# Token-number copies moved behind the weight loads of the last stage, and one register load replaced by an addition

## The reference, cut to what matters

```
x = attention(q, k, v, w_phi)                    # [2304, 512]
e = argmax(x @ w_gate); gate = softmax(...)[e] * sigmoid(x @ w_output_gate)[e]
x = gate * (relu(x @ w1[e]) @ w2[e])             # hidden width 1024
xn = x / sqrt(mean(x*x) + 1e-6) * rms_g
out = (silu(xn @ w_g) * (xn @ w_val)) @ w_out    # hidden width 1536
```

## Time and profile before

| | |
|---|---|
| median of 3 runs | 903.44 us (901.85 to 903.90) |
| profiled execution, its own time | 900.01 us |
| its span | 898.3 us |
| PE matmuls busy | 875.0 us, 97% of the span |
| PE weight loads busy | 794.5 us, 88% |
| DVE, ACT, POOL busy | 430.7, 294.0, 123.0 us |
| experts' steps | about 211 to 436 us |
| FFN | about 436 to 896 us |

### The profile page before, as it was taken

One profiled execution on the slowest core, in us unless ns is written; L12 is line 12 of the kernel. 1 busy time (PEld: TensorE's weight loads), 2 busy tenths in 40 slices (PEclk: granted clock), 3 DMA queues, 4 the chain that ended last, 5 costly groups with the idle time before them and its releaser, 6 DMA issues.

```text
span 898.3 us, 16710 instructions
## 1 busy us (share of the span) xinstructions
PE 875.0 (97%) x6432; PEld 794.5 (88%) x6433; DVE 430.7 (48%) x875; ACT 294.0 (33%) x479; POOL 123.0 (14%) x145
## 2 busy tenths in 40 slices
PE   8999999999999999999899999999999999999996
PEld 6776859588999999999899999999999999999996
DVE  5688888997587434443456422222222222222222
ACT  4555545652356333222444321121121112112111
POOL 1010203033234221125200010010000001001001
PEclk9999999999999999999999999999999999999998
DMA  8614614021754444328633720030020002000000
GB/s 280 201 54 176 225 53 158 2 81 40 256 149 119 80 79 65 69 30 183 153 128 119 178 88 1 1 106 1 1 70 35 0 25 80 0 0 36 1 1 36
DMA packets 37185, 75.37 MB, mean 84 GB/s; under 512 B 8176, under 2 KB 24688, under 8 KB 35472
## 3 DMA queue, kind: packets, MB, share of 16 engines
q1 hardware_dynamic: 32832, 56.07, 23.5%
q0 software_dynamic: 3488, 17.85, 5.4%
q10 hardware_dynamic: 816, 0.79, 0.3%
HBM read 51.06 MB, written 23.64 MB: 83 GB/s over the span
## 4 chain that ended last, share of the span: by engine, by line
PE 85%; DVE 8%; issue 3%; ACT 2%; DMA 1%; POOL 0%; DVEq 0%; POOLq 0%; SPq 0%; ACTq 0%
PE ps L1025 11%; PE ps L1027 10%; PE ps L1026 10%; PE ps L1040 5%; PE ps L1041 5%; PE ps L1039 5%; PE ps L927 4%; PE ps L928 4%; PE ps L929 4%; PE ps L940 3%; PE ps L942 3%; PE ps L941 3%; PE ps L768 3%; PE ps L823 2%; PE ps L728 2%
## 5 line engine op out<-in xcount | busy, mean ns | idle before, releaser
L1025 PE MATMUL ps<-xnH,blkH 128*128 128x384 f32 x576 | 194.6, 338 | 3.3 <-DVE blkL L1692 2.3
L1027 PE MATMUL ps<-xnH,blkL 128*128 128x384 f32 x576 | 194.2, 337 | 0.0
L1026 PE MATMUL ps<-xnL,blkH 128*128 128x384 f32 x576 | 194.1, 337 | 0.0
L1699 DVE TENSOR_TENSOR sg<-sg,ps 128x384 f32<-128x384 f32 x72 | 39.9, 554 | 246.6 <-ACT sg L1258 246.6
L1258 ACT ACTIVATE sg<-ps 128x384 f32<-128x384 f32 x72 | 35.4, 491 | 253.2 <-PE ps L1027 253.2
L1025 PEld LDWEIGHTS ps<-xnH,blkH 128*128 128x128 f32 x576 | 108.8, 189 | 7.5 <-issue 4.7
L1026 PEld LDWEIGHTS ps<-xnL,blkH 128*128 128x128 f32 x576 | 108.9, 189 | 2.7
L1027 PEld LDWEIGHTS ps<-xnH,blkL 128*128 128x128 f32 x576 | 108.8, 189 | 0.0
L1040 PE MATMUL ps<-blkL,hH 128*128 128x512 f32 x216 | 84.9, 393 | 0.0
L1041 PE MATMUL ps<-blkH,hL 128*128 128x512 f32 x216 | 84.8, 393 | 0.0
L1039 PE MATMUL ps<-blkH,hH 128*128 128x512 f32 x216 | 84.6, 391 | 0.0
(11 more groups left out here) (219 smaller groups left out, 1552.5 us busy)
## 6 DMA issues: line engine op xcount, KB each, us to landing
stage<-in_ffn_w SPq DMA_DIRECT2D x12, 768.0 KB, 4.3
xin<-xs_dram SPq DMA_DIRECT2D x9, 578.2 KB, 9.9
xs_dram<-zrow SPq DMA_DIRECT2D x8, 578.2 KB, 8.0
qT<-in_q SPq DMA_DIRECT2D x4, 1152.0 KB, 6.5
xnH_dram<-xoH SPq DMA_DIRECT2D x8, 576.0 KB, 3.5
xnL_dram<-xoL SPq DMA_DIRECT2D x8, 576.0 KB, 4.9
xnH<-xnH_dram SPq DMA_DIRECT2D x6, 768.0 KB, 4.9
xnL<-xnL_dram SPq DMA_DIRECT2D x6, 768.0 KB, 6.3
```

The lines of the kernel that those rows point to most:

```text
L1025: e.matmul(o, hi, xnH[par][:, c, :], start=(c == 0), stop=False)
L1026: e.matmul(o, hi, xnL[par][:, c, :], start=False, stop=False)
L1027: last = e.matmul(o, lo, xnH[par][:, c, :], start=False, stop=(c == KC - 1))
```

## The change

In SP's program `rows_out` is cut in two. The stores of the rows stay; the copy of the token numbers becomes `numbers_out`, with the load of the row number that only it needs. In the loop it is called right behind `rows_out`. For the last two steps both copies stand behind the loads of all weight blocks and behind the last step's row stores, ahead of the wait for `xst` and of `group_in(1)`. In `over_turns` the first step of a pair's second turn is the sum of the first turn's two numbers, in place of a load.

```
+        def tiles_of(e, x):
+            return e.value_load(tab[0:1, bass.ds(x + TILES, 1)], min_val=0, max_val=NTOK // G)
...
-                    tiles, first = turn_of(e, pair * 2 + par)
+                    if par == 0:
+                        tiles, first = turn_of(e, pair * 2)
+                    else:
+                        first = first + tiles
+                        tiles = tiles_of(e, pair * 2 + 1)
...
             def rows_out(n):
-                col, row = column_of(n), row_of(n)
+                col = column_of(n)
                 e.wait_ge(s["act_xh"], n + 2)
...
                 e.dma_start(xnL_dram[:, :, bass.ds(col, G)], xoL[:, :, :].bitcast(F32)).then_inc(s["xst"], 16)
+
+            def numbers_out(n):
+                col, row = column_of(n), row_of(n)
                 e.wait_ge(s["idst"], n * 16 + 16)
                 settle(e, "carry_sp")
                 with nc.allow_non_contiguous_dma(reason="token numbers"):
...
             with e.Fori(0, total - 2) as n:
                 rows_next(n + 2)
                 rows_out(n)
+                numbers_out(n)
             rows_next(total)
...
             for i in range(3, NF):
                 block_in(i)
             rows_out(last)
+            numbers_out(prior)
+            numbers_out(last)
             e.wait_ge(s["xst"], total * 32 + 64)
             settle(e, "carry_sp")
             group_in(1)
```

More of the change, by code:

```diff
@@ L345, in piece_of, with tiles_of @@
             return w1[:, n, :] if n < KC else w2[:, 2 * (n - KC):2 * (n - KC) + 2, :].rearrange("p c n -> p (c n)")
+        def tiles_of(e, x):
+            return e.value_load(tab[0:1, bass.ds(x + TILES, 1)], min_val=0, max_val=NTOK // G)
         def turn_of(e, x):
-            tiles = e.value_load(tab[0:1, bass.ds(x + TILES, 1)], min_val=0, max_val=NTOK // G)
+            tiles = tiles_of(e, x)
             first = e.value_load(tab[0:1, bass.ds(x + FIRST, 1)], min_val=0, max_val=NTOK // G + E)
```

## The result

| | kernel before | changed kernel |
|---|---|---|
| median | 903.31 us (901.85 to 903.90, 4 runs) | 913.44 us (912.52 to 914.60, 4 runs) |
| ratio to before | | 1.011, 95% interval 1.0094 to 1.0126 |
| profiled execution, its own time | 900.01 us | 914.60 us |
| its span | 898.3 us | 913.0 us |

The change makes the kernel 10.1 us slower. I had forecast 4.0 us slower, with a range up to 910.0: the direction was right, the size was not, and the time lies above the range. In the lines of the changed kernel L1025 to L1027 of before are L1040 to L1042, L1692 is L1707, L533 is L546, L513 is L526, L498 is L510 and L518 is L531.

A forecast was written before the change was run, and what follows sets the result against it. PE was taken as the bound, 85% of the chain. Block 2 -3.7, register loads -1.0, stall +7.0 and clock +1.7 summed to +4.0 us, from a median of 903.44 to 907.4 us, range 900.5 to 910.0.

The forecast's parts named there:

- Part 3: Loop: row number loaded between stores and copy delays copy and `xin` load about 1.1 us, hidden by transposes; cost nothing.
- part 1: Block 2's load without a copy ahead lands earlier: 1.98 us of PE idling and 1.70 of slow clock go, gain 3.7.
- Part 4: Both copies ahead of group 1's rows: PE stalls 7.0 us, plus 1.7 us of slow clock behind it.
- (b): Bound on group 1's stall: row stores' own transfer is part of the first copy's time; rows land 520.6, stall 5.5 us.
- rival 3: Block 2's load is late because of the seam's row stores, not the copy; stall stays, +7.7, 911.1 us; chance 0.06.
- Part 2: Load of `first` goes twice on PE, ahead of the second and empty fourth turns: gain 1.0 us (0 to 1.4).
- Part 5: DVE waits for `idF` at group 0's end; 3.3 us are spare, so nothing unless rows are in time and `idF` late.
- rival 1: Copies ahead of group 1's rows are quick, no stall, only the gains stay: -4.7, 898.7 us; chance 0.15.

The follow-up runs named there:

- r3: The kernel before with only the seam changed: both last copies behind the last row stores, ahead of group 1's rows; 909.79 us, ratio 1.0073.
- r5: The kernel before with only the copy of the last step but one moved behind block 3's load; 895.79 us against 897.20, ratio 0.9986.
- r7: The changed kernel with the loop of before, both numbers loaded ahead of the row stores; 903.40 us against 897.20, ratio 1.0070.
- r10: The changed kernel with the loop of before and the last copy behind group 1's rows; 900.00 us against 902.47, ratio 0.9974.
- r4: The kernel before with only the loop changed: both numbers loaded again between row stores and copy; 904.58 us, ratio 1.0020.
- r6: The changed kernel with one line moved: the last step's copy goes behind group 1's rows; 896.90 us, ratio 0.9991.
- r12: r4 with two more register loads on POOL ahead of the issue of the second turn's `w2`; ratio 1.0023.
- r1: The kernel before, unedited, run and profiled again; 903.29 us, ratio 1.0004.
- r2: The kernel before with only the register load of `first` replaced by an addition; median 902.72 us against 902.34.
- r8: r4 with one more pair of register loads ahead of each copy; 901.96 us against 897.20, ratio 1.0046.
- r9: r4 with the column number kept in its register, only the row number loaded between stores and copy; 902.24 us, ratio 0.9999.
- r11: r5 with the changed register loads added; 899.65 us against 902.47, ratio 0.9973.

## Why the prediction went wrong, by its own steps

Two terms were wrong. Part 3 put the loop at nothing, and it costs about 1.8 us; part 1 put the gain at block 2 at 3.7 us, and it is 1.3 by the clock. The register loads may hold up to 1.6 us more. The stall, the largest term, was right.

**Part 4, the stall: right.** Forecast: second copy some 8 us behind the first, rows 1 us behind that, stall 7.0 (5.5 to 9.3) plus 1.7 for the clock. Measured: 8.2 us, 0.8 us, an idle time of 7.7, 5.8 and 5.0 us in three kernels, and 9.5, 8.3 and 6.7 us in the parts with the clock. The first copy took the 7.9 us of bound (b) and the row loads landed 13.9 to 15.0 us behind the second, where (b) had 520.6-506.5=14.1. The first copy itself left 504.78-499.08=5.7 us behind the end of the last weight load's issue, where the prediction had 4.7; with the 0.9 us by which its rows landed later than in (b) this accounts for most of 7.7 us against 5.5. By time, r3 against r5 gives 0.87% or 7.8 us, r7 against r10 0.96% or 8.6 us. The 2 us of fixed cost that the Trainium skill gives for the GpSimd path in DMA: Bandwidth & Descriptors, section "Anatomy of one DMA", are not what these copies on SP's queue take: 7.9 us with nothing queued behind it. The Trainium skill, DMA: Bandwidth & Descriptors, section "Rules for kernel authors", says that a copy whose last dimension is strided becomes one descriptor for each element. The trace agrees: of packets under 512 bytes it counts 305 from 506.0 to 512.9 us, when the first copy was nearly alone, and 304 from 514 to 516, behind the second's issue; that is one for each of the 288 numbers and 16 or 17 more.

**Part 3, the loop: this step failed.** "That load is for a step that starts over 20 us later, whose transposes hide it: nothing." The cover was there for the rows, but I looked at the rows alone and not at what was being loaded beside them. The two loads (not one) between store and copy put the row load 1.6 us later against `w2`'s, its lead was gone, and both landed late; `w2` has no cover, since ACT waited 1.16 us for it already in before. The ratios make it +1.8 us in r4 and 1.5 in r10 against r6. The step had no term for the clock either, and in the profiles a slow stretch of 1.7 us is part of the price. That lead and landing go together is shown by r12; why `w2` too lands later when the rows come beside it and not ahead is only argued. Why it landed late in r3, which had the lead, is open; but r3's steps 2 and 3 then cost what those of r4 cost, so they go by the landing of `w2`, whatever made it late.

**Part 1, block 2: mechanism right, size too large.** The load takes 4.4 us instead of 10.07 and the wait is gone, so rival 3 is out. The forecast of 3.7 us is the 22.31-18.6 of the table to 0.1 us. But the six other profiles that keep the copy in front of block 2's load (r1, r2, r4, r8, r9, r12) show 19.5 to 21.2 us there, all at a clock of 1.00. The term that was mis-sized is the 1.70 us of clock, taken from one execution, and r5 gives the whole gain as 1.3 us.

**Part 2, the register loads: idle time right, gain smaller.** Of PE's idle time 0.47 and 0.8 us went, as the rows said; the first came back in step 2, which waits for `w2` and not for PE. The step "I take half a us each" took each idle time as one that sets the end. What is left in time lies between +0.6 us (r2) and -1.2 (r11 against r5), so neither a gain nor none is shown.

**Part 5: right.** `idF` came late, and no wait of PE came of it, with DVE waiting 4.8 us in r6; in the changed kernel it waited 7.5, under PE's stall.

**The sum.** Forecast -3.7-1.0+8.7+0=+4.0. By the timed runs: block 2 -1.3, register loads between +0.6 and -1.2, stall about +8.2, loop about +1.8: +7.5 to +9.3, against +10.1 (8.5 to 11.4). Of the 6.1 us that the forecast was short, 2.4 are block 2, 1.8 the loop, and up to 1.6 the register loads; the stall gives 0.5 back. What is left lies within the intervals. Rival 1 needed both copies and the rows within 16.5 us of the first issue; it took 8.2 us to the second issue and 15.0 from there.

## What to carry to other kernels

A small strided copy is dear by its latency: put it where nothing that somebody waits for stands behind it in the queue, and never two that wait for each other in a row. Before a delay on a transfer queue is called hidden, list what other large transfers are issued within 2 us of it, and look whether one of them has no slack; here an order that flipped by 1.7 us made both land later. Look at the granted clock behind each wait that grows, not at the wait alone. And a cost that is seen in one profiled execution (a slow clock, a wait) is a term of the sum only if a second profile has it too.

## What the runs showed that I had not expected

A copy of 288 numbers of 4 bytes, 1.1 KB, took 6.7 to 10.5 us to landing in the eleven profiles that time it, with row stores ahead or without (r6's second: 9.65 us from its issue at 506.13 until `idF` could go). For the last 4.7 of the first copy's 7.9 us in the changed kernel the DMA engines' share was 0.00, so there it is neither bytes nor other traffic. What the time is spent on is not shown.

The same 2 us of idling at the same place was followed by 3.4 us at half clock in one profile of the kernel before and by full clock in the other; the 5.0 to 7.7 us of idling were followed by half clock in the three profiles that have them. At the end of step 2 the same was seen in six of six profiles behind 2.1 to 2.5 us of idling, and in none of the eight with 0.3 to 1.7. So a wait that grew by 0.3 us, from r2's to r12's, came with 1.7 us more. The length alone doesn't decide it: block 2's 2.3 us in r1 were followed by full clock.
